# A fused attention, token-mixer and channel-mix kernel: first batch's low x moved to GpSimd, second token-up tile by chunks, six weight splits moved and halved, step 0 of the next batch prepared earlier

## Chip, cores and metric

One core of a Trainium2 chip (trn2). The metric is the device time of one launch in microseconds, the median of the runs. Engines: TensorE (PE), VectorE (DVE), ScalarE (ACT), GpSimd (POOL), and the DMA queue of SyncE (SP).

## What is computed

Four batches, eight heads, 768 positions, 48 features a head, so that x is 768 by 384 per batch. Per batch:

```python
state = alpha[:, :, t, :, None] * state + einsum('bhd,bhe->bhde', k[:, :, t], v[:, :, t])
y[:, :, t] = einsum('bhd,bhde->bhe', q[:, :, t], state)        # attention -> x
h = maximum(x.T @ w_tok1, 0) @ w_tok2;  u = x + h.T             # token mixer, d_tok 256
x2 = u + maximum(u @ w_ch1, 0) @ w_ch2                          # channel mixer, d_ch 1536
xk, xr = mu * x2 + (1 - mu) * shifted(x2)                       # for mu_k and mu_r
out = sigmoid(xr @ w_r) * (maximum(xk @ w_k, 0) ** 2 @ w_v)     # d_ff 1024
```

## The kernel before

**Number form.** Most products are made from pairs of fp32r tiles, a high part and a low part (value minus high part), in three passes: high by high, high by low, low by high. ScalarE writes a high part and VectorE or GpSimd the low part. This holds for x, h, u, the hidden tiles, q and k from the second batch on, and for every weight.

**Attention.** A batch is 24 steps: 6 chunks of 128 positions by 4 pairs of heads. A step turns q, k and alpha, scans alpha forward and backward (L1017, L1019), scales q and k (L1026 to L1034), forms scores, masks them, and forms y (128 by 96) and the update of the pair's state (L1062, L1065), from which GpSimd clears the blocks between two heads (`own_head`, L455). y becomes x: ScalarE copies it to `x[0]` (L839, `high_x`), VectorE subtracts for `x[1]` (L1070, in `outputs`), and GpSimd adds both into `x_sum` once per chunk (L462, `add_x`, 128 by 384).

**The order.** Every engine has its order written out by hand in slots, 28 per batch (`SLOTS`). In the first batch (the head) slot s holds the transposes of step s, the scores of step s-2 and the output of step s-3. The first batch's attention runs alone; then attention of batch r runs in the slots of the mixer of batch r-1 (`for r in range(1, B)`), and a last pass mixes batch 3. `prepared_in(s)` says which step is prepared in slot s of a batch: step 0 in slot 0 and step s-1 in slots 2 to 24; scores come one slot after it, the output two, the copies of the output three.

**The mixer's slots.** Slot 0 is the second token-up tile (`token_up(b, 1)`, 18 matmuls, L655; the first tile is made after the slots of the batch before, in the head in six chunks of three matmuls by `early_token_up`, L666). Slots 1 to 3 are two token-down tiles each (L677 transposes, L686). From slot 4 (`FIRST_UNIT`) each slot makes one hidden tile (`channel_up`, L698, 9 matmuls) and adds the one before into the sums (`channel_down`, L714, 9 matmuls). All tiles pass through two banks; `claim` waits until the low part of the tile two before has been taken. The high parts of the tiles are L866, the low ones L1100 and L1102. The low parts of q (`split_low`, L1044) read two tiles in SBUF. `read_sums` (L1110) adds the sums to `x2_half`, which GpSimd prepares from u (L482) in slots 8 to 13 and stores (L487); at the end of a batch it waits for its stores (`finish_stores`).

**Weights.** A weight piece of 128 by 768 is loaded by SP into one of three raw buffers (L356), copied high by ScalarE (L814, `split_hi`) and subtracted low by GpSimd (L448, `split_lo`). `PIECES` 0 to 3 are w_tok1 and w_tok2, 4 to 9 w_ch1, 10 to 15 w_ch2. `pieces_in(s)` spreads the first 13 over slots 5 to 27 of the head. The last three are split by GpSimd alone in slots 4, 6 and 8 of the next batch (`split_late`: L521 then L448). `channel_down` waits for the piece of w_ch2 that it needs. In the head the output of step i also waits (`attention_out`) until the low x of step i-2 is written, which frees its bank.

After the mixers comes the channel mix (L764, L773, L786) in a loop over half batches. The change doesn't touch it.

## Time and profile before

| | |
|---|---|
| median of 3 runs | 758.2 us (757.63 to 758.41) |
| the profiled execution's own time | 757.72 us |
| its span, first to last instruction | 756.0 us |
| PE busy | 740.8 us (98%), 4598 matmuls |
| DVE, ACT, POOL busy | 469.6 (62%), 327.6 (43%), 188.9 us (25%) |
| chain that ended last | PE 87%, DVE 7%, ACT 2%, issue 2%, DMA 1% |
| matmul lines with the most of the chain | L698 19%, L714 19%, L786 13%, L764 12% |
| mean granted TensorE clock | 0.993 of full |

A busy share is an average over stages. A matmul's modelled end lies some 0.16 us behind the start of the next one, so a gap on PE is that much longer than the idle time that the profile shows. A line's start and length in the timeline cover all instructions that it merges. "issue" as releaser means that the profile shows no event; the wait is then read from the program's waits.

### The profile page before, as it was taken

Reading aid. Unit: us, or ns where it says so; the run is one execution under the profiler, and the core shown is the slowest. Engines: PE = TensorE matmul, PEld = TensorE weight load, DVE = VectorE, ACT = ScalarE, POOL = GpSimd, SP = SyncE. Lnnn points to the kernel's source line nnn. Section 1 sums busy time; section 2 is a strip of 40 time slices with the busy share of each in tenths; the row PEclk is TensorE's granted clock in tenths of the full one; section 3 lists DMA queues with packets and bytes.
Section 4 is the critical chain, followed back from the end, with each engine's and each line's share of the span. In section 5 each row is a group of like instructions: output and inputs, shape, how many; then the busy total and the mean of one; then the engine's idle time right before and its main releaser. Section 6 shows DMA issues by size and latency. Waiting matters only on the chain.

```text
span 756.0 us, 13704 instructions
## 1 busy us (share of the span) xinstructions
PE 740.8 (98%) x4598; PEld 727.7 (96%) x4598; DVE 469.6 (62%) x1307; ACT 327.6 (43%) x915; POOL 188.9 (25%) x318
## 2 busy tenths in 40 slices
PE   8999999999999999999999999999899999999998
PEld 7888899999999999899999999999899999999998
DVE  6986997863877873787875221436374473563651
ACT  4664444441544442444444131236273363463541
POOL 1783563342244333135325250001000000000000
PEclk9998999999999999999999999999999999999999
DMA  9874333341232432134340024010010110110000
GB/s 201 191 143 122 49 44 51 68 57 44 34 50 37 87 40 40 46 43 59 69 81 2 33 71 149 33 32 31 32 33 32 52 42 32 42 52 31 10 21 31
DMA packets 174026, 43.81 MB, mean 58 GB/s; under 512 B 161296, under 2 KB 171152, under 8 KB 173968
## 3 DMA queue, kind: packets, MB, share of 16 engines
q1 hardware_dynamic: 170720, 37.98, 25.3%
q0 software_dynamic: 1152, 4.72, 1.7%
q8 instruction: 30, 0.49, 0.3%
q10 hardware_dynamic: 2096, 0.39, 0.3%
q14 instruction: 28, 0.23, 0.1%
HBM read 33.63 MB, written 9.44 MB: 57 GB/s over the span
## 4 chain that ended last, share of the span: by engine, by line
PE 87%; DVE 7%; ACT 2%; issue 2%; DMA 1%; POOL 0%; SPq 0%; DVEq 0%; ACTq 0%
PE bank L698 19%; PE bank L714 19%; PE bank L786 13%; PE bank L764 12%; PE bank L773 4%; PE bank L616 4%; PE bank L594 3%; PE bank L686 3%; PE bank L655 2%; PE bank L620 2%; PE bank L623 1%; DVE qs_lo L1044 1%; PE bank L677 1%; PE bank L589 1%; DVE decays L1017 1%
## 5 line engine op out<-in xcount | busy, mean ns | idle before, releaser
L866 ACT ACTIVATE hid_hi<-bank 128x384 fp32r<-128x384 f32 x96 | 47.2, 492 | 116.5 <-PE bank L698 116.4
L1100 DVE SCALAR_TENSOR_TENSOR hid_lo<-bank,hid_hi 128x384 fp32r<-128x384 f32 x96 | 53.3, 555 | 70.3 <-ACT hid_hi L866 67.1
L959 ACT ACTIVATE relu_k<-bank 128x384 f32<-128x384 f32 x64 | 31.5, 493 | 102.7 <-PE bank L764 85.0
L698 PE MATMUL bank<-u_hi,wch_hi 128*128 128x384 f32 x288 | 71.9, 357 | 1.5 <-issue 1.5
L698 PE MATMUL bank<-u_lo,wch_hi 128*128 128x384 f32 x288 | 65.9, 336 | 0.0
L714 PE MATMUL bank<-hid_lo,wch_hi 128*128 128x384 f32 x288 | 65.6, 335 | 0.0
L698 PE MATMUL bank<-u_hi,wch_lo 128*128 128x384 f32 x288 | 65.5, 334 | 0.0
L714 PE MATMUL bank<-hid_hi,wch_hi 128*128 128x384 f32 x288 | 65.4, 334 | 0.0
L714 PE MATMUL bank<-hid_hi,wch_lo 128*128 128x384 f32 x288 | 65.3, 334 | 0.0
L1216 DVE TENSOR_TENSOR x_half<-bank,x_half 128x384 f32<-128x384 f32 x24 | 13.4, 558 | 77.4 <-PE bank L786 77.4
L839 ACT ACTIVATE x_hi<-bank 128x96 fp32r<-128x96 f32 x96 | 23.6, 246 | 84.9 <-PE bank L623 67.2
L468 POOL TENSOR_SCALAR_AFFINE_SELECT relu_k<-relu_k 128x256 f32<-128x256 f32 x72 | 29.6, 412 | 120.2 <-ACT relu_k L848 120.2
L1044 DVE SCALAR_TENSOR_TENSOR qs_lo<-qkd,rhead,qs_hi 96x128 fp32r<-96x128 f32 x144 | 52.3, 402 | 10.8 <-ACT qs_hi L860 7.7
L1199 DVE TENSOR_TENSOR relu_k<-relu_k 128x384 f32<-128x384 f32 x64 | 35.7, 558 | 27.9 <-ACT relu_k L959 24.3
L698 PEld LDWEIGHTS bank<-u_lo,wch_hi 128*128 128x128 f32 x288 | 51.7, 188 | 0.0
L698 PEld LDWEIGHTS bank<-u_hi,wch_lo 128*128 128x128 f32 x288 | 51.5, 188 | 0.0
L714 PEld LDWEIGHTS bank<-hid_hi,wch_hi 128*128 128x128 f32 x288 | 51.2, 188 | 0.1
L714 PEld LDWEIGHTS bank<-hid_hi,wch_lo 128*128 128x128 f32 x288 | 51.3, 188 | 0.0
L714 PEld LDWEIGHTS bank<-hid_lo,wch_hi 128*128 128x128 f32 x288 | 51.3, 188 | 0.0
L473 POOL TENSOR_TENSOR ks_lo<-qkd,ks_hi 96x128 fp32r<-96x128 f32 x72 | 33.1, 460 | 66.2 <-ACT ks_hi L856 58.2
L698 PEld LDWEIGHTS bank<-u_hi,wch_hi 128*128 128x128 f32 x288 | 47.1, 190 | 2.2 <-issue 2.0
L860 ACT ACTIVATE qs_hi<-qkd,rhead 96x128 fp32r<-96x128 f32 x144 | 49.0, 388 | 0.0
(122 smaller groups left out, 1827.3 us busy)
## 6 DMA issues: line engine op xcount, KB each, us to landing
w_raw<-in_moe_w_ch SPq DMA_DIRECT2D x12, 384.0 KB, 3.5
x_scratch<-x_half POOLq DMA_DIRECT2D x8, 576.0 KB, 3.5
out<-x_half SPq DMA_DIRECT2D x24, 192.0 KB, 1.9
vt<-in_v SPq DMA_DIRECT2D x48, 72.0 KB, 2.2
qka<-in_q SPq DMA_DIRECT2D x49, 48.0 KB, 2.2
qka<-in_alpha SPq DMA_DIRECT2D x49, 48.0 KB, 2.2
qka<-x_scratch SPq DMA_DIRECT2D x4, 577.5 KB, 3.8
qka<-in_k SPq DMA_DIRECT2D x48, 48.0 KB, 2.2
```

What stands on the lines that cost most here:

```text
L473: nc.gpsimd.tensor_tensor(ks[1][0:W2, i % 2, :], qkd[0:W2, second_of(i), :], ks[0][0:W2, i % 2, :], ALU.subtract)\
L616: mm = nc.tensor.matmul(y_ps[:, h * D:(h + 1) * D], am[:, i % 2, h * P:(h + 1) * P], v_of(r, i)[:, h * D:(h + 1) * D], start=(h == 0), sto ...
L698: mm = nc.tensor.matmul(dst, ch1_w(a, n % KC, jj), u[c][:, n % KC, half * HT:(half + 1) * HT], start=(n == 0), stop=(n == 3 * KC - 1))
L714: mm = nc.tensor.matmul(b_acc[m][:, 0:HT], ch2_w(a, jj, m), hid[c][:, j % HJ, :], start=(jj == 0 and n == 0), stop=(jj == NJ - 1 and n == 2))
L764: mm = nc.tensor.matmul(dst, wk_w(a, n % KC, j), mix_out[0][c][:, n % KC, :], start=(n == 0), stop=(n == 3 * KC - 1))
L786: mm = nc.tensor.matmul(bank[m][:, 0:DM], k2[a][:, n % NF, m * P:(m + 1) * P], wv_w(c, n % NF), start=(n == 0), stop=(n == 3 * NF - 1))
L860: nc.scalar.activation(dst[0:W2, h * P:(h + 1) * P], qkd[0:W2, first_of(i), :], ACT.Copy, scale=rhead[0:W2, i % 4, h:h + 1])\
L866: nc.scalar.activation(dst, b_ring[t % 2][:, 0:HT], func).then_inc(tile_hi, 1)
L959: nc.scalar.activation(relu_k[:, j % 2, :], b_ring[j % 2][:, 0:HT], ACT.Relu)\
L1044: nc.vector.scalar_tensor_tensor(qs[1][0:W2, i % 2, cols], qkd[0:W2, first_of(i), :], rhead[0:W2, i % 4, h:h + 1], qs[0][0:W2, i % 2, cols ...
L1100: ins = nc.vector.scalar_tensor_tensor(dst, src, 0.0, hi, ALU.max, ALU.subtract)
L1199: nc.vector.tensor_tensor(relu_k[:, j % 2, :], relu_k[:, j % 2, :], relu_k[:, j % 2, :], ALU.mult).then_inc(k2_ready, 1)
```

## The change

The first batch's low x is made by GpSimd: ScalarE copies y twice, in full to `x_sum` and rounded to `x[0]`, GpSimd subtracts per step (`low_x`), and `add_x` is left out there. TensorE's output of step i in the head waits for the high x and the state of step i-2 in place of the low x. The second token-up tile of batch 0 is made in chunks in slots 24 to 26 of the head and after it. The head takes ten weight pieces, in slots 4, 6, ... 22. The six pieces of w_ch2 are copied high by ScalarE in slots 0, 2, ... 10 of the second batch, and subtracted low by GpSimd in halves of 384 columns in slots 1 to 12. Step 0 of a batch is prepared in slot 26 of the batch before (in the head: in its last slots), step 1 in slot 1, steps 2 to 23 in slots 3 to 24 as before. The first token-up tile is evicted before the last sums are read. In slots under 4 VectorE takes the low parts of tiles ahead of the scaling of q and k. The preparation of x2 moves to slots 13 to 18, and the wait for its stores to its first instruction of the next batch. SP loads the last three pieces between the loads of the second batch's third half.

```diff
-    BASE_SLOT = 2 * FIRST_UNIT
+    BASE_SLOT = NJ + 1
+        def lo_count(n):
+            return n if n <= CH1_END else 2 * min(n, NMIX) - CH1_END + max(n - NMIX, 0)
         def pieces_in(s):
-            bounds = [max(n - (SLOTS - STEPS), 0) * NEARLY // STEPS for n in (s, s + 1)]
+            bounds = [min(max(n - 3, 0) * CH1_END // (STEPS - NP), CH1_END) for n in (s, s + 1)]
-        def prepared_in(s):
-            if s == 0:
-                return 0
-            return s - 1 if 2 <= s <= STEPS else None
+        def step_in(s, lag):
+            n = s - lag
+            if n in (-1, 1):
+                return max(n, 0)
+            return n - 1 if 3 <= n <= STEPS else None
+        def prepared(r, s):
+            if s == SLOTS - 2:
+                return (r + 1, 0) if r + 1 < B else None
+            i = step_in(s, 0)
+            return None if i is None else (r, i)
...
+            def split_half_lo(jj):
+                n, half = divmod(jj, 2)
+                _, dst, off = PIECES[CH1_END + n]
+                cols = slice(off + half * DM, off + (half + 1) * DM)
+                pool.wait_ge(w_hi_ready, CH1_END + n + 1)
+                nc.gpsimd.tensor_tensor(dst[1][:, cols], staging(CH1_END + n)[0][:, half * DM:(half + 1) * DM],
+                                        dst[0][:, cols], ALU.subtract).then_inc(w_lo_ready, 1)
+            def low_x(i):
+                c, p = step(0, i)
+                xs = slice(p * W2, (p + 1) * W2)
+                pool.wait_ge(xhi_ready, i + 1)
+                nc.gpsimd.tensor_tensor(x[1][:, c, xs], x_sum[:, c, xs], x[0][:, c, xs], ALU.subtract)\
+                    .then_inc(xlo_ready, 1)
...
+            def batch_slot(r, s):
+                sc, yo, prep = step_in(s, 2), step_in(s, 3), prepared(r, s)
                 if sc is not None:
                     clear_future(r, sc)
+                if r == 1 and 1 <= s <= NJ:
+                    split_half_lo(s - 1)
                 if yo is not None and step(r, yo)[0] < NC - 1:
                     own_head(r, yo)
                 if yo is not None and step(r, yo)[1] == NP - 1:
                     add_x(r, step(r, yo)[0])
+                if BASE_SLOT <= s < BASE_SLOT + 2 * KC:
+                    prepare_x2(r - 1, s - BASE_SLOT)
+                if prep is not None:
+                    split_k(*prep)
...
-                    pe.wait_ge(xlo_ready, i - 1)
+                    pe.wait_ge(xhi_ready, i - 1)
+                    pe.wait_ge(state_sum, min(i - 1, NST))
...
-                    early_token_up((s - 2) // NP - 2)
-            early_token_up(NC - 1)
+                    early_token_up((s - 2) // NP - 2, 0)
+                if STEPS <= s <= STEPS + 2:
+                    for c in range(2 * (s - STEPS), min(2 * (s - STEPS) + 2, NC - 1)):
+                        early_token_up(c, 1)
+            for m in range(KT):
+                early_token_up(NC - 1, m)
...
+                if prep is not None:
+                    spread_q(*prep)
+                if r == 1 and s % 2 == 0 and s < NJ:
+                    split_hi(CH1_END + s // 2)
             def high_x(r, i):
+                if is_first(r):
+                    nc.scalar.activation(x_sum[:, c, p * W2:(p + 1) * W2], y_kv(r, i)[0], ACT.Copy)
...
+                if s == STEPS + 1:
+                    scale_qk(1, 0)
                 if yo is not None:
                     outputs(0, yo)
+                if s == STEPS:
+                    turn(1, 0)
+                    scans(1, 0)
             def batch_slot(r, s):
...
+                if 0 < s < FIRST_UNIT:
+                    tile_first(r - 1, s)
+                if prep is not None:
+                    scale_qk(*prep)
+                if s >= FIRST_UNIT:
+                    tile_first(r - 1, s)
+                if s < FIRST_UNIT:
+                    tile_second(r - 1, s)
+                if prep is not None:
+                    split_low(*prep)
...
+            split_low(1, 0)
+            tile_first(0, 0)
             for r in range(1, B):
                 for s in range(SLOTS):
                     batch_slot(r, s)
+                tile_first(r, 0)
                 read_sums(r - 1, 1)
```

## Rows read from the trace of the kernel before

**Rows 1.** Stretches: length, busy PE, PEld, DVE, ACT, POOL, granted clock, DMA share, GB/s

```profile
18.37:24.24 5.87, 5.77 (x44) 4.86 (x43) 5.76 (x25) 3.94 (x14) 5.46 (x6) 1.00 0.81 183
24.24:51.07 26.83, 26.22 (x200) 23.48 (x198) 26.38 (x109) 18.67 (x60) 20.44 (x25) 1.00 0.84 186
51.07:54.80 3.73, 2.81 (x19) 2.29 (x17) 2.71 (x10) 2.68 (x7) 3.47 (x4) 1.00 0.61 72
54.80:61.60 6.80, 6.80 (x23) 6.67 (x24) 2.42 (x9) 2.27 (x5) 3.44 (x3) 0.50 0.82 214
...
77.45:178.59 101.14, 99.53 (x659) 98.37 (x658) 77.78 (x233) 43.20 (x149) 46.13 (x81) 1.00 0.35 51
178.59:200.75 22.16, 21.08 (x135) 20.00 (x135) 14.61 (x43) 7.79 (x23) 3.39 (x7) 1.00 0.18 40
200.75:299.39 98.64, 98.64 (x660) 98.11 (x658) 72.03 (x233) 43.59 (x149) 38.03 (x75) 1.00 0.36 53
```

**Rows 2.** Timeline of PE, slots 10 to 13 of the head: start, length

```profile
24.24 0.54 PE L616 MATMUL bank<-vt,relu_k 128*128 128x48 f32 x4
...
26.48 0.54 PE L616 MATMUL bank<-mixed,relu_k 128*128 128x48 f32 x4
...
28.24 0.54 PE L616 MATMUL bank<-mixed,relu_k 128*128 128x48 f32 x4
...
29.05 0.25 PE L585 MATMUL bank<-ident,qkd 96*128 96x96 f32 x1
29.38 0.70 PE L589 MATMUL bank<-x_half,qkd 96*128 96x256 f32 x2
```

**Rows 3.** Timeline of DVE over one step of the head

```profile
26.91 0.44 DVE L1051 COPY_PREDICATED relu_k<-causal,bank 128x256 f32<-128x256 uint32 x1
...
27.57 0.39 DVE L1019 TENSOR_TENSOR_SCAN decays<-bank,mixed 96x127 f32<-96x127 f32 x1
...
28.74 0.25 DVE L1070 TENSOR_TENSOR x_lo<-bank,x_hi 128x96 fp32r<-128x96 f32 x1
28.91 0.43 DVE L1051 COPY_PREDICATED relu_k<-causal,bank 128x256 f32<-128x256 uint32 x1
...
29.57 0.39 DVE L1019 TENSOR_TENSOR_SCAN decays<-bank,mixed 96x127 f32<-96x127 f32 x1
```

**Rows 4.** Groups by form from 18 to 50 us

```profile
L448 POOL TENSOR_TENSOR wtok_lo<-w_raw,wtok_hi 128x768 fp32r<-128x768 f32 x4 | 7.3, 1813 | 2.7 <-ACT wtok_hi L814 2.7
...
L455 POOL TENSOR_TENSOR state<-state,own 96x96 f32<-96x96 f32 x16 | 6.2, 386 | 2.2 <-DVE state L1065 2.2
...
L839 ACT ACTIVATE x_hi<-bank 128x96 fp32r<-128x96 f32 x17 | 4.0, 238 | 0.0
...
L462 POOL TENSOR_TENSOR x_sum<-x_hi,x_lo 128x384 f32<-128x384 f32 x4 | 4.0, 999 | 0.0
```

**Rows 5.** Timeline of PE, the head's last slots and the first token-down tile

```profile
53.47 0.67 PE L589 MATMUL bank<-x_half,qkd 96*128 96x256 f32 x2 [0.69 <-ACT x_half L860]
...
65.20 0.44 PE L686 MATMUL bank<-wtok_hi,h_lo 128*128 128x384 f32 x1 [0.97 <-DVE h_lo L1100]
```

**Rows 6.** Timelines of DVE, POOL and PE in the second batch, one split

```profile
78.89 2.62 DVE L1044 SCALAR_TENSOR_TENSOR qs_lo<-qkd,rhead,qs_hi 96x128 fp32r<-96x128 f32 x2 [0.63 <-ACT qs_hi L860]
...
79.53 1.83 POOL L448 TENSOR_TENSOR wch_lo<-w_raw,wch_hi 128x768 fp32r<-128x768 f32 x1
...
81.61 0.35 PE L594 MATMUL bank<-qs_hi,ks_hi 96*128 96x256 f32 x1 [0.68 <-issue]
```

**Rows 7.** Timeline of PE, the passage from batch to batch

```profile
187.14 0.52 PE L677 MATMUL bank<-ident,x_sum 128*128 128x128 f32 x3 [0.59 <-issue]
...
197.89 0.76 PE L698 MATMUL bank<-u_hi,wch_hi 128*128 128x384 f32 x3 [0.50 <-issue]
```

**Rows 8.** The page's groups that evict the tiles: busy, mean ns, idle before

```profile
L866 ACT ACTIVATE hid_hi<-bank 128x384 fp32r<-128x384 f32 x96 | 47.2, 492 | 116.5 <-PE bank L698 116.4
L1100 DVE SCALAR_TENSOR_TENSOR hid_lo<-bank,hid_hi 128x384 fp32r<-128x384 f32 x96 | 53.3, 555 | 70.3 <-ACT hid_hi L866 67.1
```

More of the change, by code:

```diff
@@ L384, in _ @@
                 for n in pieces_in(s):
-                    if n + NRAW < NMIX:
-                        load_piece(n + NRAW)
+                    load_piece(n + NRAW)
             for r in range(1, B):
                 for n in range(2 if r == 1 else 0, HALVES):
+                    if r == 1 and n == 2:
+                        load_piece(NMIX - 3)
                     load_half(r, n)
+                    if r == 1 and n == 2:
+                        load_piece(NMIX - 2)
                     load_half_v(r, n)
+                    if r == 1 and n == 2:
+                        load_piece(NMIX - 1)
             for n in range(NMIX, NALL):
@@ L458, in add_x @@
             def add_x(r, c):
-                if c == 0 and not is_first(r):
+                if c == 0:
                     pool.wait_ge(tile_done, TILES * (r - 1) + KT + 2 * KC)
-                pool.wait_ge(xlo_ready, NP * (c + 1) if is_first(r) else STEPS * (r + 1) - NC + c + 1)
+                pool.wait_ge(xlo_ready, STEPS * (r + 1) - NC + c + 1)
                 nc.gpsimd.tensor_tensor(x_sum[:, c, :], x[0][:, c, :], x[1][:, c, :], ALU.add).then_inc(x_sum_ready, 1)
@@ L480, in prepare_x2 @@
                 us = slice(half * HT, (half + 1) * HT)
+                if m == 0 and b > 0:
+                    pool.wait_ge(x2_stored[half], 16 * b)
                 pool.wait_ge(tile_lo, TILES * b + KT + n + 3)
@@ L488, in store_x2 @@
                                x2_half[half][:, :, :]).then_inc(x2_stored[half], 16)
-            def finish_stores(b):
-                for half in range(2):
-                    pool.wait_ge(x2_stored[half], 16 * b + 16)
             def head_part(s):
                 _, _, yo = head_steps(s)
-                if yo is not None and step(0, yo)[0] < NC - 1:
-                    own_head(0, yo)
-                if yo is not None and step(0, yo)[1] == NP - 1:
-                    add_x(0, step(0, yo)[0])
-            def attention_part(r, s):
-                sc, yo = prepared_in(s - 2), prepared_in(s - 3)
+                if yo is not None:
+                    low_x(yo)
+                    if step(0, yo)[0] < NC - 1:
+                        own_head(0, yo)
+            def batch_slot(r, s):
+                sc, yo, prep = step_in(s, 2), step_in(s, 3), prepared(r, s)
                 if sc is not None:
                     clear_future(r, sc)
+                if r == 1 and 1 <= s <= NJ:
+                    split_half_lo(s - 1)
                 if yo is not None and step(r, yo)[0] < NC - 1:
@@ L514, in _ @@
                     split_lo(n)
-            def split_late(n):
-                _, dst, off = PIECES[n]
-                rows, cols = piece_size(n)
-                raw, loaded, value = staging(n)
-                pool.wait_ge(loaded, value)
-                nc.gpsimd.tensor_copy(dst[0][:, off:off + rows * cols], raw).then_inc(w_hi_ready, 1)
-                split_lo(n)
+            split_k(1, 0)
             for r in range(1, B):
                 for s in range(SLOTS):
-                    attention_part(r, s)
-                    if BASE_SLOT <= s < BASE_SLOT + 2 * KC:
-                        prepare_x2(r - 1, s - BASE_SLOT)
-                    if prepared_in(s) is not None:
-                        split_k(r, prepared_in(s))
-                    late, odd = divmod(s - FIRST_UNIT, 2)
-                    if r == 1 and odd == 0 and 0 <= late < NMIX - NEARLY:
-                        split_late(NEARLY + late)
+                    batch_slot(r, s)
                     if s == FIRST_UNIT + NJ:
@@ L673, in token_down @@
                 dst = claim(b, t)
-                if m == 0:
-                    pe.wait_ge(x_sum_ready, NC * b + TM * (half + 1))
+                if m == 0 and b > 0:
+                    pe.wait_ge(x_sum_ready, NC * (b - 1) + TM * (half + 1))
                 for n in range(TM):
@@ L1058, in outputs @@
                 y_ps, kv_ps = y_kv(r, i)
+                if is_first(r) and c == NC - 1:
+                    return
                 dve.wait_ge(xhi_ready, G + 1)
@@ L1068, in outputs @@
                     ins.then_inc(state_sum, 1)
+                if is_first(r):
+                    return
                 xs = slice(p * W2, (p + 1) * W2)
@@ L1175, in _ @@
                     batch_slot(r, s)
+                tile_first(r, 0)
                 read_sums(r - 1, 1)
```

56 lines of the change are left out of this document (28 added, 28 removed).

## The prediction, made before the change was run

> **What bounds the kernel now.** The chain that ended last is TensorE for 87%, and the engine is busy 98% of the span, so time comes back only where TensorE stands still, waits behind modelled ends, or runs at a low clock. I read the stretches first. From 200.75 to 299.39, slots 5 to 27 of the third batch, TensorE is busy for all of 98.64 us [rows 1]. The same slots of the second batch take 101.14 us for the same matmuls: 2.50 us of waits. The passage from 178.59 to 200.75 has 1.08 us of idle time, the head's last slots (51.07 to 54.80) have 0.92 us, and the 6.80 us after them are granted 0.50 of the clock, the lower of the two levels (1.2 GHz), after an engine that had stood still in two slots [rows 1].
>
> Then the timelines. In the head VectorE makes one step in 26.91 to 28.91, 2.00 us, without a gap, and its last 0.17 us (28.74 to 28.91) are the low x [rows 3]. TensorE is close behind: its slots take 2.24 us with a token-up chunk and 1.76 us right after one (24.24, 26.48, 28.24); in the others a matmul of L589 starts 0.33 us behind L585 where 0.09 would do, waiting for q and k [rows 2]. In the second batch a whole-piece split of 1.83 us on GpSimd lies over the two low parts of q on VectorE, which take 2.62 us together; TensorE's scores stand still for them at 81.61 [rows 6].
>
> **The change, part by part.**
>
> *Head pace.* VectorE loses the low x: 2.00 - 0.17 = 1.83 us a step [rows 3]. TensorE then sets the pace: four slots take 4 x 1.76 + 0.48 for the chunk = 7.52 us, 1.88 a slot [rows 2]. Slots 11 to 23 took 26.2 us and would take about 24.8 (the four chunks among them): 1.4 us. The three slots before, without a chunk, go from 5.87 [rows 1] to 3 x 1.83: 0.4 us. The slots before those gain 0.2. Sum 2.0 us. ScalarE adds one copy per step, 0.24 us by its twin L839 [rows 4]; it is busy 18.67 of 26.83 us [rows 1], so this is hidden, and with that cover gone it would cost 0.24 x 20 = 4.8 us. The state's update comes that copy later, but its result is read four steps on.
>
> GpSimd's low x isn't in the trace. Its nearest row is the 96 by 96 product at 0.39 us, which has the same 96 columns; the upper bound is the 384-column sum at 1.00 us [rows 4]. I take 0.39. Over two slots (3.76 us) GpSimd has one split, 1.81, two state products, 0.78, and two low x, 0.78: 3.4 us, and the sum per chunk (L462) is gone. Splits take one slot in two, against 13 in 24 before. Behind a split wait the state products, with three slots of slack, the low x, with four slots until a chunk of token-up reads them, and SP's next raw load. The loads of the next batch's first half stand behind that in SP's queue; they began near 40 us before, and the piece ahead of them is split one slot earlier, so they still land well ahead of slot 24, where VectorE would otherwise hold up the last masks.
>
> *End of the head.* Fifteen matmuls of the second token-up tile move into slots 24 to 26. Before, TensorE waited there 0.92 us, plus 0.16 behind each of two waits: 1.2 us [rows 1, 5]. With 0.17 a matmul at full clock, the 2.6 us of moved work fills all of it. A busy engine keeps its clock: up to 51.07 the granted clock was full with waits of 0.24 in most slots [rows 1, 2]. The 6.80 us at half clock become 3.4. The wait at 65.20 for h's low part, 0.97 + 0.16, came from GpSimd's last head splits, which are gone: 1.1 us [rows 5]. Slot 4's wait for VectorE (0.50 + 0.16; the twin of 197.89) goes, since slots 1 to 3 have one preparation less and u's low part comes ahead of the scaling [rows 7]. A new wait appears: the two h tiles now end 0.5 us apart, and eviction of the first takes 0.49 on ScalarE, 0.56 on VectorE and some 0.25 for handing over [rows 8], 1.3 us, against 1.0 us of matmuls left (a chunk and the scores): 0.3. Sum 1.2 + 3.4 + 1.1 + 0.65 - 0.3, rounded down: 6.0 us.
>
> *Splits in the second batch.* Twelve half pieces, not in the trace: half of 1.81 is the lower bound, the 384-column sum at 1.00 the upper, which I take since it has the same shape [rows 4]. A half split comes right behind the mask, when VectorE transposes and scans, and is over some 1.5 us before the low part of q starts; the state product behind it is late by 1.0 us, where TensorE reads it some 2 us later. ScalarE's three extra 0.83 us copies come behind its last job of a slot and delay the next high x by 0.5 us, within the same slack. So slots 5 to 27 fall to the 98.64 of the third batch: 2.5 us [rows 1].
>
> *Passages into the third and fourth batch.* Step 0 is made in slot 26, where VectorE is half idle, the first h tile is evicted before the sums, and the scores of step 0 stand ahead of token-down. The waits at 187.14 and 197.89 go: 0.59 + 0.50 and 0.16 behind each [rows 7], with 0.1 for a small one between: 1.5 us. Two such passages: 3.0 us. The third passage, into the last mixer pass, has no attention beside it and stays.
>
> *The rest.* Preparing x2 moves to slots 13 to 18, four slots before the sums need its last tile; the store's wait is asked a batch later. The three late raw loads on SP each wait for a half split, one or two slots before their neighbours' own waits come true. No cost. The channel mix isn't touched.
>
> Sum: 2.0 + 6.0 + 2.5 + 3.0 = 13.5 us. The profiled execution took 757.72 us with a span of 756.0, 0.5 under the median of 758.2. I forecast 744.2 for the like, 744.7 as median.
>
> **A rule that speaks against it.** VectorE's scan at 27.57 lies wholly under a GpSimd split and takes 0.39 us; at 29.57, with GpSimd idle for most of it, it takes 0.39 too [rows 3]. So in the head, where VectorE reads at most one full tile from SBUF, I let GpSimd's new work cost VectorE nothing. The Trainium skill (Perfetto Trace Analysis, Optimizing Scalar/DVE Operations) warns that GpSimd and VectorE share an SBUF read port, "so offloading operations between those two might not help". The rows of the head disagree; the row of L1044, with two SBUF inputs, agrees.
>
> **The rivals.**
>
> 1. *The clock still falls.* TensorE's output in slot 26 needs a mask, an eviction and GpSimd's low x in a row. If it stands still as long as before, the stretch at half clock stays: 3.4 us less gain, 748.1 us. For it: that chain is longer by one engine. Against it: 1.1 us of matmuls lie beside it. 0.10.
>
> 2. *Half splits still block the low part of q.* The three whole splits cost 2.5 us for 5.5 us of split. If twelve halves at 1.0 cost in proportion, that is 5.5 us, so 744.7 + 5.5 = 750.2. Against: their place in the slot. 0.08.
>
> 3. *The head keeps VectorE's pace* by handovers between four busy engines: 2.0 us lost, 746.7 us. 0.12.
>
> 4. *GpSimd's work blocks VectorE in the head.* Each low x would hold VectorE 0.39 us: 2.22 a step, 0.22 over before for 20 steps, and the 2.0 is lost: 744.7 + 6.4 = 751.1. This is the cited rule's case. Rows 3 speak against it. 0.03.
>
> 5. *Slower: GpSimd becomes the head's pace.* Above (3.76 - 2.59) / 2 = 0.59 us per low x it does; at the bound of 1.00 two slots take 4.59 us, 0.42 a slot over 1.88 for 19 slots, 7.9 us: 752.6. To pass 759.7 the price must give back 15 us: 0.79 a slot, a low x of 1.4 us, more than the row of four times its columns. 0.03 for slower, 0.02 for the part short of it.
>
> 6. *The waits only change places,* nothing comes of it but the moved work: 758.2. 0.02.
>
> **How the numbers follow.** The forecast, 743 to 746 us, has 0.60. The rivals have the rest. From 742 to 750.5 lie the forecast, rivals 1 and 3, most of rival 2, and bounds such as a low x of up to 0.7 us or a stretch of low clock at 532 us that comes out shorter or longer. Faster or slower by over 0.2% (1.5 us) is about what a measurement here can tell from no change: faster 0.95, within 0.2% 0.02, slower 0.03.
>
> **What would show it.** After: head steps near 1.88 us on PE and VectorE no longer without gaps; L462 three quarters as often (18 times) and a new GpSimd line at 0.39 us; no stretch at half clock from 50 to 60 us; L1044 near 0.35 us on average; slots 5 to 27 of the second batch near 98.7 us; the passages 1.5 us shorter; TensorE's busy time down by about 5 us, most of it from the clock. It would be wrong if the low clock or a wait at the h tiles stays, if low x takes over 0.6 us, or if waits of L594 on L1044 appear beside half splits.

## The result, and the profile after

The changed kernel takes 746.29 us in the median (744.92 to 747.21), the kernel before beside it 758.24 us (757.63 to 758.41): a ratio of 0.9844 [0.9824, 0.9865], 11.9 us less. The forecast was 744.7 us in a range of 742.0 to 750.5; the narrower 743 to 746 us, which had a chance of 0.60, was missed by 0.3. The profiled execution took 746.56 us with a span of 744.8; by the spans the gain is 11.2 us, and the shares below are of these 11.2. Two of the kernels further down had one execution each that took over 11 us longer at a mean granted clock of 0.98, and the medians given leave it out.

Lines of the page of the changed kernel: its span, the busy times, the chain that ended last, and the group of q's low parts.

```profile
span 744.8 us, 13733 instructions
...
PE 735.3 (99%) x4598; PEld 725.2 (97%) x4598; DVE 462.3 (62%) x1283; ACT 333.1 (45%) x942; POOL 189.3 (25%) x339
...
PE 92%; DVE 3%; ACT 3%; issue 1%; DMA 1%; SPq 0%; DVEq 0%; ACTq 0%
...
L1079 DVE SCALAR_TENSOR_TENSOR qs_lo<-qkd,rhead,qs_hi 96x128 fp32r<-96x128 f32 x144 | 46.6, 362 | 10.3 <-ACT qs_hi L891 6.6
```

The chain is TensorE for 92% (87% before), and the engine is busy 5.5 us less for the same 4598 matmuls. 3.4 us of this is the stretch at half clock that is gone; the rest is put down to gaps, each of which lengthens a modelled end by some 0.16 us. The other 5.7 us of the gain were gaps themselves.

The windows view of the changed kernel answers to [rows 1]. Columns: stretch, its length, busy time and count on PE, PEld, DVE, ACT and POOL, granted clock, DMA share, GB/s.

```profile
24.29:31.92 7.63, 7.57 (x61) 6.89 (x60) 7.36 (x29) 6.14 (x24) 6.40 (x11) 1.00 0.88 199
...
50.11:58.38 8.27, 8.12 (x52) 7.44 (x51) 5.08 (x17) 4.61 (x18) 4.01 (x7) 1.00 0.66 118
58.38:71.33 12.95, 12.54 (x86) 12.18 (x86) 11.38 (x28) 7.65 (x21) 6.01 (x9) 1.00 0.37 82
71.33:170.75 99.42, 98.93 (x658) 98.09 (x657) 75.47 (x244) 46.88 (x155) 46.29 (x84) 1.00 0.39 60
170.75:191.29 20.54, 20.54 (x135) 20.33 (x135) 12.14 (x33) 7.17 (x21) 3.13 (x7) 1.00 0.18 41
191.29:289.96 98.67, 98.67 (x659) 98.08 (x658) 74.97 (x242) 44.27 (x152) 38.11 (x76) 1.00 0.36 53
```

Four head slots now take 7.63 us (24.29 to 31.92). The head's end and the first token-down tiles run at a clock of 1.00, where 6.80 us had been granted 0.50 before [rows 1]. Slots 5 to 27 of the second batch take 99.42 us and not yet the 98.67 of the third. The passage takes 20.54 us, against 22.16 [rows 1], without a gap.

Measured between the same matmuls in both traces, the 11.2 us lie as follows. Later tables use the same cuts.

| stretch | before | after |
|---|---|---|
| start to slot 3 of the head | 11.11 | 11.71 |
| slot 3 to slot 23 | 39.32 | 37.76 |
| slot 23 to the first token-down tile | 12.44 | 9.07 |
| from there to slot 5 of the second batch | 16.25 | 14.38 |
| slots 5 to 27 and into the third batch's token-up | 99.47 | 97.83 |
| passage into the third batch | 23.83 | 22.13 |
| passage into the fourth | 23.81 | 22.12 |
| the last mixer pass and the channel mix | 316.01 | 315.94 |

The first row isn't the change's. It differs between executions of kernels with the same start (10.33 to 11.91 us in the runs of this study), and part of such a delay is still there in slot 23: 0.72 us of 1.25 between the two traces of the changed kernel.

What is left of waits from 58 to 78 us, by the waits view of the changed kernel (engine and line, what it waited for, us in total, times, longest):

```profile
PE bank L604 <- ACT relu_k L881: 0.5, 1, 0.5
PE bank L698 <- DVE h_lo L1151: 0.3, 1, 0.3
PE bank L613 <- issue: 0.2, 1, 0.2
```

L1151 is the handover of the second h tile, which the prediction had. The two others it had not. Their neighbours in the timelines of PE, DVE, POOL and ACT (start, length, idle before) of the changed kernel:

```profile
62.78 1.50 DVE L1079 SCALAR_TENSOR_TENSOR qs_lo<-qkd,rhead,qs_hi 96x128 fp32r<-96x128 f32 x2
62.87 1.00 POOL L472 TENSOR_TENSOR wch_lo<-w_raw,wch_hi 128x384 fp32r<-128x384 f32 x1
...
69.28 1.51 DVE L1079 SCALAR_TENSOR_TENSOR qs_lo<-qkd,rhead,qs_hi 96x128 fp32r<-96x128 f32 x2
69.38 1.01 POOL L472 TENSOR_TENSOR wch_lo<-w_raw,wch_hi 128x384 fp32r<-128x384 f32 x1
70.90 0.36 PE L613 MATMUL bank<-qs_hi,ks_hi 96*128 96x256 f32 x1 [0.25 <-issue]
...
73.76 0.83 ACT L840 ACTIVATE wch_hi<-w_raw 128x768 fp32r<-128x768 f32 x1
74.76 0.23 ACT L881 ACTIVATE relu_k<-bank 128x96 f32<-128x96 f32 x1
...
75.14 0.27 PE L604 MATMUL bank<-ident,qkd 96*128 96x96 f32 x1 [0.49 <-ACT relu_k L881]
```

Two half splits did not come behind a mask but over q's low parts, which took 1.50 us in place of their usual 0.61 (below), and TensorE stood still for 0.25 + 0.16 us at 70.90. And ScalarE's copy of a weight piece held up its copy of the transposed k (L881) out of the bank that TensorE's next transpose of k (L604) writes: 0.49 + 0.16 us at 75.14.

### The profile page after: what moved, and what is told of

It is laid out like the page before. It is cut to its first block, busy times and chain, and to the rows that moved or that the text cites. A ratio compares the mean times of both kernels' runs of the same rounds, so it can differ in the third digit from the quotient of the medians.

```text
span 744.8 us, 13733 instructions
## 1 busy us (share of the span) xinstructions
PE 735.3 (99%) x4598; PEld 725.2 (97%) x4598; DVE 462.3 (62%) x1283; ACT 333.1 (45%) x942; POOL 189.3 (25%) x339
## 3 DMA queue, kind: packets, MB, share of 16 engines
HBM read 33.63 MB, written 9.44 MB: 58 GB/s over the span
## 4 chain that ended last, share of the span: by engine, by line
PE 92%; DVE 3%; ACT 3%; issue 1%; DMA 1%; SPq 0%; DVEq 0%; ACTq 0%
PE bank L719 20%; PE bank L735 20%; PE bank L812 14%; PE bank L790 12%; PE bank L799 4%; PE bank L636 4%; PE bank L613 4%; PE bank L707 3%; PE bank L675 3%; PE bank L640 2%; PE bank L643 2%; PE bank L698 1%; PE bank L608 1%; PE bank L604 1%; PE bank L585 1%; PE bank L687 1%
## 5 line engine op out<-in xcount | busy, mean ns | idle before, releaser
L1151 DVE SCALAR_TENSOR_TENSOR hid_lo<-bank,hid_hi 128x384 fp32r<-128x384 f32 x96 | 53.3, 555 | 68.3 <-ACT hid_hi L897 65.0
L719 PE MATMUL bank<-u_hi,wch_hi 128*128 128x384 f32 x288 | 71.7, 357 | 0.0
L719 PE MATMUL bank<-u_lo,wch_hi 128*128 128x384 f32 x288 | 65.9, 336 | 0.0
L719 PE MATMUL bank<-u_hi,wch_lo 128*128 128x384 f32 x288 | 65.4, 334 | 0.0
L1079 DVE SCALAR_TENSOR_TENSOR qs_lo<-qkd,rhead,qs_hi 96x128 fp32r<-96x128 f32 x144 | 46.6, 362 | 10.3 <-ACT qs_hi L891 6.6
L719 PEld LDWEIGHTS bank<-u_lo,wch_hi 128*128 128x128 f32 x288 | 51.7, 188 | 0.0
L719 PEld LDWEIGHTS bank<-u_hi,wch_lo 128*128 128x128 f32 x288 | 51.5, 188 | 0.0
L636 PE MATMUL bank<-vt,relu_k 128*128 128x48 f32 x352 | 47.6, 257 | 0.0
L636 PEld LDWEIGHTS bank<-vt,relu_k 128*128 128x128 f32 x352 | 47.2, 191 | 0.0
```

What stands on the lines that cost most here:

```text
L636: mm = nc.tensor.matmul(y_ps[:, h * D:(h + 1) * D], am[:, i % 2, h * P:(h + 1) * P], v_of(r, i)[:, h * D:(h + 1) * D], start=(h == 0), sto ...
L719: mm = nc.tensor.matmul(dst, ch1_w(a, n % KC, jj), u[c][:, n % KC, half * HT:(half + 1) * HT], start=(n == 0), stop=(n == 3 * KC - 1))
L1079: nc.vector.scalar_tensor_tensor(qs[1][0:W2, i % 2, cols], qkd[0:W2, first_of(i), :], rhead[0:W2, i % 4, h:h + 1], qs[0][0:W2, i % 2, cols ...
L1151: ins = nc.vector.scalar_tensor_tensor(dst, src, 0.0, hi, ALU.max, ALU.subtract)
```

## The experiments

Three things were to be tested: the low x is what lets the head go at TensorE's pace; the chunks keep the clock up; the order and place of small jobs in slots 0 to 12 of the second batch explain both the gain there and the waits that stay. Each kernel is the changed one with one edit, but for the last two, which build on the one before them. Stretches are compared between the same matmuls, as in the table. The changed kernel run again had 745.93 us (744.22 to 747.75) beside 757.38 before, a ratio of 0.9851 [0.9834, 0.9867], and gives a second set of stretches: slot 23 at 48.75 us, then 9.07, 14.35, 97.83, 22.09, and 314.44 for the last part. The intervals of six of the kernels below overlap that of the changed kernel (low x on VectorE, low x twice, the second tile in slot 0, the old order, whole splits, half splits behind the state). Their medians alone don't separate them from it; what is read from them rests on the stretches of one trace each.

> The changed kernel once more, as it is. Theory (what varies from run to run is when TensorE's clock is first granted in full, and whether it falls after the 2.2 us wait for the last weights near 520 us): the times spread over 2 to 3 us; the stretches between 60 and 500 us agree with the first profile to 0.1 us; the start differs by up to 1.4 us and the last stretch is either 314.4 or 316.0 us.

### Low x back on VectorE

```diff
                 if yo is not None:
-                    low_x(yo)
...
-                    pe.wait_ge(xhi_ready, i - 1)
-                    pe.wait_ge(state_sum, min(i - 1, NST))
+                    pe.wait_ge(xlo_ready, i - 1)
...
-                if is_first(r) and c == NC - 1:
-                    return
...
-                if is_first(r):
-                    return
```

> The changed kernel with the head's low x back on VectorE (0.17 us a step) and GpSimd without it; ScalarE keeps its two copies. Theory (VectorE's 2.00 us a step set the head's pace, and the low x is what it lost): four head slots take 8.0 us again in place of 7.63, the output of slot 23 comes 1.6 us later, the whole 1.5 to 2.0 us above the changed kernel. Rival (the pace came from fewer or later weight splits, or from the looser wait of TensorE): four slots stay at 7.6 to 7.7 us and the time stays within 0.5 us.

Measured: 747.67 us (746.22 to 748.39), ratio 0.986 [0.9834, 0.9886]. Slot 23 starts at 50.38 us, 1.63 later than in the changed kernel run again. From slot 3 to slot 23 it takes 39.80 us against 38.29, 1.51 more; the rest is a start 0.12 us later. The timeline of DVE has the step of [rows 3] again:

```profile
28.69 0.25 DVE L1103 TENSOR_TENSOR x_lo<-bank,x_hi 128x96 fp32r<-128x96 f32 x1
28.86 0.44 DVE L1084 COPY_PREDICATED relu_k<-causal,bank 128x256 f32<-128x256 uint32 x1
...
30.69 0.25 DVE L1103 TENSOR_TENSOR x_lo<-bank,x_hi 128x96 fp32r<-128x96 f32 x1
30.86 0.43 DVE L1084 COPY_PREDICATED relu_k<-causal,bank 128x256 f32<-128x256 uint32 x1
```

2.00 us from mask to mask, without idle time on VectorE. So the head's pace comes from this one instruction's place, and it is worth 1.5 us. The edit also gives TensorE back its wait for the low x of step i-2. That wait wasn't tested by itself; the VectorE step without a gap speaks for the instruction. Slots 5 to 27 of the second batch take 0.30 us more, with a wait of 0.80 us at L603 where the changed kernel has 0.49 at L604; why isn't known.

### A second low x per step on GpSimd

```diff
                 pool.wait_ge(xhi_ready, i + 1)
+                spare = u[1][:, :, :].rearrange("p c t -> p (c t)")[:, i * W2:(i + 1) * W2]
+                nc.gpsimd.tensor_tensor(spare, x_sum[:, c, xs], x[0][:, c, xs], ALU.subtract)
                 nc.gpsimd.tensor_tensor(x[1][:, c, xs], x_sum[:, c, xs], x[0][:, c, xs], ALU.subtract)\
...
```

> The changed kernel with GpSimd's low x of the head made twice, once into unused space: 0.35 us more per step. Theory (GpSimd has 0.3 us a slot to spare, 0.59 us per low x is where it starts to set the pace): two slots cost GpSimd 1.8 + 0.7 + 1.4 = 3.9 us against 3.82, so the head is longer by 0.5 to 1.5 us. Rival (GpSimd's waits for its operands add to its work, it is the pace already): longer by the whole 0.35 x 20 = 7 us, or nearly. Other rival (nothing waits for it): under 0.2 us.

The extra instruction writes where nothing is read. Measured: 745.24 us (745.19 to 745.29), ratio 0.9824 [0.9801, 0.9848]: no loss that a median shows. In the stretches only slot 23 to the first token-down tile is longer, 9.44 us against 9.07, with one wait of 0.2 us for the low x. GpSimd's timeline over two slots of this kernel:

```profile
24.00 1.84 POOL L463 TENSOR_TENSOR wtok_lo<-w_raw,wtok_hi 128x768 fp32r<-128x768 f32 x1
25.78 0.41 POOL L481 TENSOR_TENSOR u_lo<-x_sum,x_hi 128x96 fp32r<-128x96 f32 x1
26.13 0.41 POOL L482 TENSOR_TENSOR x_lo<-x_sum,x_hi 128x96 fp32r<-128x96 f32 x1
26.48 0.41 POOL L489 TENSOR_TENSOR state<-state,own 96x96 f32<-96x96 f32 x1
...
27.87 1.83 POOL L463 TENSOR_TENSOR wtok_lo<-w_raw,wtok_hi 128x768 fp32r<-128x768 f32 x1
```

It runs without a gap at 3.87 us for two slots against the 3.82 that TensorE takes (7.63 / 2), and the head keeps its pace: 37.81 us from slot 3 to slot 23, 37.76 in the changed kernel. By start times two low x take 0.70 us a step (26.48 less 25.78), a little over the forecast's threshold of 0.59, and that fits: GpSimd falls behind by 0.05 us in two slots, which shows as 0.37 us at the end of the head, between the expectation's 0.5 to 1.5 us and the under 0.2 of its rival. VectorE wasn't slowed by a GpSimd that never rests: from 24 to 50 us its scans take 412 and 392 ns on average, 411 and 391 in the changed kernel.

### The second token-up tile in slot 0 again

```diff
                 if s == 0:
-                    if b > 0:
-                        token_up(b, 1)
+                    token_up(b, 1)
...
-                if STEPS <= s <= STEPS + 2:
-                    for c in range(2 * (s - STEPS), min(2 * (s - STEPS) + 2, NC - 1)):
-                        early_token_up(c, 1)
-            for m in range(KT):
-                early_token_up(NC - 1, m)
+            early_token_up(NC - 1, 0)
```

> The changed kernel with the second token-up tile of batch 0 as 18 matmuls in slot 0 of the second batch, not in chunks. Theory (the chunks fill waits of 1.2 us and keep the clock up, which was worth 3.4 us): TensorE waits about 1 us between 50 and 55 us, the granted clock falls to 0.50 for 6.8 us, and the stretch from slot 24 to slot 4 is longer by 1.2 + 3.4 less the 0.4 us wait for h: 4.2 us above the changed kernel. Rival (the low clock came from the weight splits at the end of the head and is gone without the chunks): the clock stays up and only 0.5 to 1.2 us are lost.

Measured: 747.36 us (746.50 to 748.33), ratio 0.9859 [0.9827, 0.9891]. The stretch from slot 23 to the first token-down tile takes 11.13 us, 2.06 more than with chunks. Windows of this kernel:

```profile
50.00:52.90 2.90, 2.38 (x16) 2.02 (x15) 2.78 (x10) 1.62 (x7) 2.43 (x3) 1.00 0.59 78
52.90:56.30 3.40, 3.40 (x14) 2.94 (x14) 1.34 (x6) 1.55 (x7) 1.26 (x4) 0.58 0.57 110
```

TensorE stands still for 0.52 us (a wait of L608 for ScalarE's `x_half` at 51.64), and the stretch behind it is granted 0.58 of the clock on average: it runs at 1.2 GHz for 3.41 us, 1.7 us lost. The rival (the clock stays up) falls. But the theory's 4.2 us falls too: before, the half clock lasted 6.83 us, and the gaps were 0.92. Without the chunks half of that is still gone. The next kernel shows where it went.

### Weight pieces spread to slot 27 of the head

```diff
-            bounds = [min(max(n - 3, 0) * CH1_END // (STEPS - NP), CH1_END) for n in (s, s + 1)]
+            bounds = [max(n - (SLOTS - STEPS), 0) * CH1_END // STEPS for n in (s, s + 1)]
```

> The changed kernel with the ten weight pieces of the head spread over slots 6 to 27 as the kernel before spread its own, the last one in slot 27. Theory (the wait for h's low part at 65.20 of the kernel before came from the last weight pieces of the head, on ScalarE and GpSimd): the first token-down tile starts 0.8 to 1.5 us later than in the changed kernel. Rival (it came from VectorE, which was two slots behind and had step 0 still to prepare): under 0.3 us.

Measured: 752.47 us (752.08 to 752.86), ratio 0.992 [0.9895, 0.9944]. From slot 23 to the first token-down tile it takes 13.70 us, 4.6 more than the changed kernel and longer than before, and 1.0 more behind it. The head up to slot 23 takes 0.6 more too, with a wait of 0.79 us for a low part of w_tok at 25.91. Timelines of this kernel:

```profile
58.16 0.44 PE L687 MATMUL bank<-x_hi,wtok_hi 128*128 128x384 f32 x1 [0.94 <-POOL x_lo L480]
59.59 0.84 ACT L840 ACTIVATE wch_hi<-w_raw 128x768 fp32r<-128x768 f32 x1 [3.01 <-DMA w_raw<-in_moe_w_ch]
...
63.02 0.55 PE L613 MATMUL bank<-qs_hi,ks_hi 96*128 96x256 f32 x1 [3.45 <-DVE qs_lo L1079]
```

ScalarE waits 3.0 us in its written order for a raw piece to land. Behind it stand the copies of k, of q and of the h tiles, and TensorE waits 3.45 us for q's low part. The expectation of 0.8 to 1.5 us had the sign, not the size: it counted GpSimd's time, not ScalarE's fixed order with a copy at its head that waits for a transfer. The kernel before had this wait as well, as its timeline of ScalarE shows:

```profile
59.52 0.84 ACT L814 ACTIVATE wch_hi<-w_raw 128x768 fp32r<-128x768 f32 x1 [2.92 <-DMA w_raw<-in_moe_w_ch]
```

The copies of h, k and q stood behind it there too (61.42 to 61.99). Here TensorE's granted clock was 0.55 from 62.90 to 66.50 us. So with the chunks in place, ending the pieces at slot 22 is worth more than they are: the forecast gave the fall of the clock wholly to the chunks. What each would save alone from the kernel before wasn't run.

### Step 0 prepared in its own slot 0 again

```diff
         def prepared(r, s):
+            if s == 0 and r >= 2:
+                return (r, 0)
             if s == SLOTS - 2:
-                return (r + 1, 0) if r + 1 < B else None
+                return None
```

> The changed kernel with step 0 of the third and fourth batch prepared in slot 0 of its own batch, its scores still at the end of slot 0. Theory (the passages gained 1.6 us each because step 0 was made early): TensorE waits at L613 in slot 0 for about 1.5 us in each of the two passages, 3 us above the changed kernel in all. Rival (the gain of the passages came from the order of the low parts in slots 1 to 3 and from evicting the first h tile before the sums): under 0.5 us.

Measured: 751.54 us (751.16 to 751.85), ratio 0.9908 [0.9884, 0.9933]. Each of the two passages takes 25.63 us against 22.13: 3.5 us, twice. Its timeline of PE and its windows:

```profile
179.85 0.36 PE L615 MATMUL bank<-qs_hi,ks_hi 96*128 96x256 f32 x1 [1.46 <-DVE qs_lo L1081]
```

```profile
179.50:183.00 3.50, 3.15 (x14) 3.08 (x15) 1.49 (x4) 0.53 (x2) 0.41 (x1) 0.63 0.00 0
183.00:186.00 3.00, 3.00 (x21) 3.00 (x20) 1.82 (x6) 1.67 (x5) 0.41 (x1) 0.87 0.00 0
```

The wait is 1.46 + 0.16 us, and behind it the granted clock falls: 3.41 us at the lower level, 1.7 us more. The kernel before had smaller waits there, 0.59 and 0.50, and no fall [rows 7]; which of the other edits makes this wait longer than those wasn't taken apart. So 3.5 is the price of this edit and not the change's gain, which is 1.7 us a passage. It shows that the clock can double a wait's price.

### The low parts in the old order

```diff
-                if 0 < s < FIRST_UNIT:
-                    tile_first(r - 1, s)
                 if prep is not None:
                     scale_qk(*prep)
-                if s >= FIRST_UNIT:
+                if s > 0:
                     tile_first(r - 1, s)
-                if s < FIRST_UNIT:
-                    tile_second(r - 1, s)
                 if prep is not None:
                     split_low(*prep)
-                if s >= FIRST_UNIT:
-                    tile_second(r - 1, s)
+                tile_second(r - 1, s)
```

> The changed kernel with VectorE's order in slots 1 to 3 as before: scaling, first low part of u, low part of q, second low part of u. Theory (slots 1 to 3 were too full because three preparations stood in the slots from 0 to 3 with two of them in slots 2 and 3; with step 1 in slot 1 the order alone is worth little): each passage is longer by 0 to 0.3 us, under 1 us in all. Rival (the order is what removed the wait of 0.65 us at slot 4): 0.65 us a passage, 2 us over the three.

Measured: 747.23 us (747.06 to 749.77), ratio 0.985 [0.9818, 0.9881]. The first token-down tiles to slot 5 take 15.84 us against 14.38 and each passage 0.5 us more (22.67, 22.62). The waits view of this kernel from 55 to 76 us, and its timeline of PE with the fourth token-down tile (slot 2) and the first hidden tile (slot 4):

```profile
PE bank L698 <- DVE u_lo L1148: 1.2, 1, 1.2
```

```profile
64.94 0.55 PE L698 MATMUL bank<-ident,x_sum 128*128 128x128 f32 x3 [1.18 <-DVE u_lo L1148]
...
70.39 0.77 PE L719 MATMUL bank<-u_hi,wch_hi 128*128 128x384 f32 x3
```

The new wait is in slot 2, at the transposes of a token-down tile: 1.2 us in the second batch and 0.3 in each later one, each with 0.16 behind it. Slot 4, where the kernel before waited 0.50 us (L698 there, the twin of L719), has no wait, although the order is the old one. The theory's 0 to 0.3 us a passage was too little, and the rival has near its size but not its mechanism: moving u's low part ahead of the scaling didn't remove slot 4's wait. What the new order does is spare slot 2 a wait that is there with the rest of the change in place. What removed slot 4's wait is not shown; a preparation less in slots 1 to 3 is the reason left of the two that the prediction gave. The clock stayed full behind the wait of 1.2 us. The order counts for 2.5 us in these three stretches of this trace. Slots 5 to 27 are 0.40 longer too, with 0.88 us of wait at L604 in place of 0.49, as with low x on VectorE (0.80), and can't be put down to the order.

### Whole splits in odd slots

```diff
             def split_half_lo(jj):
                 n, half = divmod(jj, 2)
+                if half:
+                    return
...
-                cols = slice(off + half * DM, off + (half + 1) * DM)
+                cols = slice(off, off + 2 * DM)
...
-                nc.gpsimd.tensor_tensor(dst[1][:, cols], staging(CH1_END + n)[0][:, half * DM:(half + 1) * DM],
-                                        dst[0][:, cols], ALU.subtract).then_inc(w_lo_ready, 1)
+                nc.gpsimd.tensor_tensor(dst[1][:, cols], staging(CH1_END + n)[0][:, 0:2 * DM],
+                                        dst[0][:, cols], ALU.subtract).then_inc(w_lo_ready, 2)
```

> The changed kernel with the six late low parts of the weights as whole pieces of 1.8 us in slots 1, 3, ... 11 in place of twelve halves. Theory (a split costs TensorE time only where it starts under the low parts of q, and it does so where no mask stands ahead of it on GpSimd, in slots 2 and 4; all odd slots have a mask): no two low parts of q take over 1.1 us in slots 2 and 4, the wait at the end of slot 4 is gone, and the stretch from the first token-down tile to slot 5's down part is 0.2 to 0.4 us shorter, the time within 0.5 us of the changed kernel. Rival (the length of a split decides, as in the kernel before): the low parts of q are blocked for up to 1.8 us again and TensorE loses 1.5 to 2.5 us over the second batch.

Measured: 746.51 us (746.26 to 746.76), ratio 0.9841 [0.9817, 0.9865]: the same as halves. The part up to slot 5 takes 13.87 us, 0.51 less, and slots 5 to 27 97.98, 0.15 more. Its timelines of POOL and DVE in slot 3, the mask ahead of them at 66.55:

```profile
66.92 1.83 POOL L474 TENSOR_TENSOR wch_lo<-w_raw,wch_hi 128x768 fp32r<-128x768 f32 x1
68.98 0.46 POOL L507 TENSOR_TENSOR ks_lo<-qkd,ks_hi 96x128 fp32r<-96x128 f32 x1 [0.22 <-ACT ks_hi L889]
69.30 0.61 DVE L1081 SCALAR_TENSOR_TENSOR qs_lo<-qkd,rhead,qs_hi 96x128 fp32r<-96x128 f32 x2
```

A split of 1.83 us behind a mask is over before q's low parts, which take 0.61 us; two of 1.0 us of which one isn't behind a mask cost more. For this length the place decides.

### Half splits behind the state, the weight copy ahead of q's copy

```diff
                 if sc is not None:
                     clear_future(r, sc)
-                if r == 1 and 1 <= s <= NJ:
-                    split_half_lo(s - 1)
                 if yo is not None and step(r, yo)[0] < NC - 1:
                     own_head(r, yo)
+                if r == 1 and 1 <= s <= NJ:
+                    split_half_lo(s - 1)
...
-                if prep is not None:
-                    spread_q(*prep)
                 if r == 1 and s % 2 == 0 and s < NJ:
                     split_hi(CH1_END + s // 2)
+                if prep is not None:
+                    spread_q(*prep)
```

> The changed kernel with GpSimd's half split behind the state product instead of ahead of it, and ScalarE's weight copy ahead of the high parts of q and k instead of behind them. Theory (the 0.4 us at the end of slot 4 come from half splits over the low parts of q, the 0.65 us at the end of slot 5 from ScalarE's copy ahead of the scores' copy): no pair of low parts of q above 0.7 us, both waits gone, from the first token-down tile to the third batch's token-up 111.1 us in place of 112.2, 1.1 us off the time. Rival (these waits come from the fuller slots 1 to 5 of VectorE itself): the same waits, the same time.

Measured: 745.21 us (744.79 to 745.34), ratio 0.9825 [0.9806, 0.9843]. The edit moves two jobs at once; the trace tells them apart. Its windows, the first token-down tile to slot 5 and slots 5 to 27:

```profile
57.99:71.88 13.89, 13.89 (x95) 13.72 (x96) 11.48 (x34) 8.61 (x24) 6.43 (x11) 1.00 0.37 65
71.88:168.95 97.07, 97.07 (x648) 96.48 (x648) 73.38 (x237) 45.66 (x153) 45.96 (x83) 1.00 0.39 61
```

And its timelines of POOL and DVE in slot 3:

```profile
66.33 1.01 POOL L472 TENSOR_TENSOR wch_lo<-w_raw,wch_hi 128x384 fp32r<-128x384 f32 x1
...
68.70 0.61 DVE L1079 SCALAR_TENSOR_TENSOR qs_lo<-qkd,rhead,qs_hi 96x128 fp32r<-96x128 f32 x2
```

TensorE is busy for every microsecond of 110.96 us; in the changed kernel the two stretches took 112.2, so 1.25 us is gained. No low part of q is longer than 0.61 us, and both waits are gone. Slots 5 to 27 of the second batch take what those of the third take, 97.07 us.

### The same, with the splits of w_v between the hidden tiles

The last stretch of all, which the change doesn't touch, holds one wait: TensorE waits 2.11 us for VectorE, which splits four weight pieces in one go. The edit spreads them over the tiles of that half pass.

```diff
+                    elif j >= 2 and j % 2 == 0:
+                        split_lo(WR_END + j // 2 - 1)
-                if first:
-                    for n in range(WR_END, NALL):
-                        split_lo(n)
```

> The kernel with GpSimd's half splits behind the state product and ScalarE's copies ahead of q and k, and also the four last low parts of the value weights on VectorE between the squares of the first half batch instead of all behind them. Theory (TensorE waits 2.2 us near 520 us for these four in a row, and the clock falls after that wait in most runs, 1.5 us): the wait is gone, the last stretch is 312.1 us in place of 314.4 or 316.0, the time 743.3 to 741.5 us in all, some 3 to 4 us under the changed kernel and the least spread. Rival (VectorE is late with the squares then and TensorE's ring of two tiles waits for it): a gain under 1 us.

Measured: 740.95 us (740.71 to 741.14) beside 757.38, ratio 0.9781 [0.9767, 0.9794]: faster than both kernels. The last stretch takes 312.18 us. The changed kernel had here, in its timeline of PE:

```profile
520.13 2.84 PE L812 MATMUL bank<-wch_hi 128*128 128x384 f32 x8 [2.11 <-DVE wch_lo L1246]
```

It has the same wait in both of its traces, and a stretch at half clock behind it in one only: 315.94 us with it, 314.44 us without. Windows behind the wait, of the one trace and of the changed kernel run again:

```profile
522.00:525.50 3.50, 3.50 (x18) 3.50 (x17) 1.64 (x3) 3.20 (x6) 0.00 (x0) 0.76 0.00 0
```

```profile
520.00:523.50 3.50, 3.50 (x22) 3.50 (x21) 2.47 (x5) 2.59 (x5) 0.00 (x0) 1.00 0.00 0
```

That is 1.5 us of difference between two executions of one kernel. Of the eleven traces that have this wait, the kernel before among them, six show the half clock behind it and five don't; neither of the two without the wait has it. Five runs of the version without it lie within 0.43 us, five of the changed kernel within 3.53. The wait isn't all of that spread: four runs of the kernel just above, which has it, lie within 0.55 us.

### The order of before, with more matmuls ahead of the head

```diff
-            WARM = (4, 2, 1, 1, 1, 1, 1)
+            WARM = (4, 4, 2, 2, 1, 1, 1)
```

> The same with four more warming matmul pairs in the first slots (slot 1: 4 in place of 2, slot 2: 2 in place of 1, and the next slot the same). Theory (the first wait of 1.2 us at 5.6 us is filled, and a TensorE without a wait gets its full clock earlier): slot 3's output at 10.0 to 10.6 us in place of 10.6 to 11.9. Rival (the clock comes at a moment of its own and the extra matmuls only stand in the way): the output of slot 3 at 11.5 us or later, up to 1 us more in all.

This is the last kernel with four more `keep_warm` matmuls in the first slots. Measured: 740.74 us (740.57 to 740.91), ratio 0.9777 [0.9762, 0.9792]; slot 3 starts at 10.37 us against 10.33. The start of 10.0 to 10.6 us that was expected came, but the kernel without the extra matmuls had it too, and the two intervals overlap: no difference. What sets the spread of the start stays open.

## Why the prediction was right, and where it was not

*Head pace* (forecast 2.0 us): right in mechanism, a little too large. Low x took 0.39 us on GpSimd (387 ns, 24 times), as taken; a load of GpSimd just over the threshold cost 0.37 us; ScalarE's extra copy was hidden. Moving it back costs 1.5 us. Four slots take 7.63 us and not 7.52: in the fourth TensorE still waits for q and k, L608 being 0.31 us behind L604 where the others have 0.09. So 0.11 of each 7.63 us is VectorE's, with its step of 1.83 us and its own handovers. The traces themselves show 1.56 us less from slot 3 to slot 23, and 0.96 with the start, which came 0.6 us later in this execution.

*End of the head* (6.0 us): 5.24 measured (3.37 and 1.87). The half clock is gone there, in both traces of the changed kernel. **The step that gave its price to the chunks failed in part:** "The 6.80 us at half clock become 3.4", with 1.2 us of gaps filled, 4.6 us for the chunks. Left out, the chunks cost 2.06 us; the earlier end of the weight pieces, which had only the wait at 65.20 in the sum (1.1 us), costs 4.6 and 1.0 when undone. Both are needed, and they overlap. The prediction put the wait at 65.20 down to GpSimd's last splits; it didn't count that ScalarE stood 2.92 us before a raw piece there, ahead of the copies of h, k and q. Slot 4's wait went as forecast, but of its two reasons the order of u's low part is refuted: the order spares slot 2 a wait instead. The wait for the second h tile was forecast at 0.3 and is 0.25 + 0.16.

*Splits in the second batch* (2.5 us): 1.64 measured. The prediction saw the 0.68 us wait for q's low parts in the kernel before, not the two others, by its waits view from 77.45 to 178.59 us:

```profile
PE bank L616 <- POOL state L455: 0.9, 2, 0.6
PE bank L594 <- issue: 0.7, 1, 0.7
```

The two waits at L616 are for the state. VectorE's low parts of q took 2.62 and 2.97 us beside the splits ahead of them (78.89 and 87.86), which is the likely reason why the state came late. **Here a step failed:** "A half split comes right behind the mask." In slots 2 and 4 there is no mask (the scores of steps 0, 1 and 2 stand in slots 1, 3 and 5), and GpSimd begins these splits right behind the k part of the slot before, which is exactly when VectorE makes q's low parts. Each of these two pairs took 1.50 us, 0.89 over 0.61, for 1.0 us of split; the second cost TensorE 0.41 us (it falls in the row above, the head's end). And "behind its last job of a slot, within the same slack" was wrong for ScalarE: the copy stands ahead of the next slot's copy of k, which had no 0.8 us to give, and TensorE waited 0.65 us. Two of the prediction's own signs of being wrong came in small: a wait beside a half split (0.25 us at L613) and one at the h tiles (0.25 us). Moving both jobs brought 0.49 + 0.76 us, and slots 5 to 27 to the 98.64 forecast by [rows 1], which is 97.07 in the cuts of the table for both batches.

*Passages* (2 x 1.5 us): 1.70 and 1.69 measured, 3.4 together. Right in size, and step 0's place is needed for it; what the first h tile's earlier eviction and the place of the scores bring by themselves wasn't run. The 0.1 for a small wait between was too little by 0.2. The 20.54 us hold no idle time at all.

*The rest*: 0.07 us, nothing. As forecast.

*The rule weighed.* Over 24 low x and a GpSimd without gaps, VectorE's scan kept 0.39 us. In the head the rule that such offloading might not help did not come true, where no instruction of VectorE's step reads two full tiles in SBUF. In the second batch the one that does, L1079, was 2.5 times as long. The Trainium skill (SBUF — State Buffer, Who interferes with whom) names this pair, a VectorE instruction with two SBUF inputs beside a GpSimd instruction that reads SBUF, and says that one with at most one SBUF input doesn't contend outside the two-port performance modes; both halves of it agree with the numbers here (0.61 to 1.50 us; 0.39 and 0.39).

*The rivals.* Rival 1, the clock falls in slot 26: no, 1.00. Rival 2, half splits block q as whole ones did: 5.5 us forecast; 0.41 us came true, for 2 splits in 12, which is the mechanism at a small size. Rival 3, the head stays at VectorE's pace: a small part of it, 0.11 us in four slots. Rivals 4, 5 and 6: no. The sum of 13.5 was missed by 2.3 us in spans: start 0.6, head pace 0.4, end of head 0.8, splits 0.9, less 0.4 gained on the passages.

## What to carry to other kernels

A small job that is cheap on its own engine is priced by what stands in that slot on the other engines: write down, for each slot that gets it, which instruction it will lie beside, slot by slot, since the first slots of a batch are not like the rest. Put work that waits for a transfer behind the copies that the critical engine needs, not ahead. And count up to 1.7 us on top of a wait at TensorE: a stretch of 3.41 us at half clock may follow it, in one execution and not in the next.

## What the runs showed that was not expected

- The length of a wait alone doesn't tell whether the clock falls. It fell behind waits of TensorE of 0.52, 1.46 and 3.45 us, each time for 3.41 us at 1.2 GHz, and in the kernel before behind one of 0.69 us for 6.83. It stayed full behind 0.49, 0.94 and 1.18 us. Behind the same 2.11 us of the changed kernel it fell in one execution and not in the other. Ahead of the 0.52 us TensorE had been thinly filled (2.38 of 2.90 us, with that wait in it); the rest is open.
- A 384-column split (1.01 us) over two low parts of q lengthens them by 0.89 us; a 768-column one of 1.83 us, with a shorter GpSimd instruction ahead of it, had lengthened them by 2.01 us [rows 6]. So VectorE loses most of the time that GpSimd's instruction takes.
- GpSimd at 100% in the head, with three small instructions a slot and a split in every second, cost 0.37 us in all.
